# A three-stage kernel with smaller first-layer units, masks behind a chunk's products, and an earlier weight load

## The reference

```python
for t in range(S):
    new_re = ar * S_re - ai * S_im
    new_im = ar * S_im + ai * S_re
    S_re, S_im = (new_re + kv, new_im)                       # kv = k[t] outer v[t]
    y[:, :, t] = np.einsum('bhd,bhde->bhe', q[:, :, t], S_re)
...
h = x @ w_in;  g = h * np.clip(h + 3.0, 0.0, 6.0) / 6.0;  x = g @ w_out
...
h = x @ w_in;  g = np.maximum(h, 0.0) + alpha * np.minimum(h, 0.0);  out = g @ w_out
```

## Time and profile before

| | us |
|---|---|
| median of 3 executions (1058.98 to 1059.59) | 1059.11 |
| the profiled execution | 1056.71 |
| its span, first to last instruction | 1055.0 |
| TensorE busy in the span | 964.5 (91%) |
| VectorE busy | 615.8 (58%) |
| ScalarE busy | 485.1 (46%) |
| GpSimd busy | 303.5 (29%) |
| TensorE's clock, mean share of full speed | 0.979 |

### The profile page before, as it was taken

The page is one execution under the profiler, slowest core; times in us unless marked ns, Lnnn a source line. Parts: engine busy times, 40 slices in busy tenths (PEclk is TensorE's granted clock), DMA queues, the critical chain, the costliest instruction groups (busy, mean ns, idle before and its releaser), DMA issues.

```text
span 1055.0 us, 16550 instructions
## 1 busy us (share of the span) xinstructions
PE 964.5 (91%) x6306; PEld 845.2 (80%) x6306; DVE 615.8 (58%) x1050; ACT 485.1 (46%) x848; POOL 303.5 (29%) x259
## 2 busy tenths in 40 slices
PE   0468888999999998889999999999999999999997
PEld 0468887999999998888787888888888888888886
DVE  6578967888888888667772244453343433433332
ACT  6467666776667776556652444221121211211111
POOL 2048311222222222111222233332332333333232
PEclk9998989999999999889999999999999999999999
DMA  6460432334323333323221701001010010010000
GB/s 199 127 177 24 99 97 69 97 77 107 98 70 91 85 88 98 90 72 78 67 56 37 269 31 60 1 1 60 1 45 16 1 60 1 22 38 1 30 1 31
DMA packets 79616, 70.46 MB, mean 67 GB/s; under 512 B 32560, under 2 KB 76592, under 8 KB 79152
## 3 DMA queue, kind: packets, MB, share of 16 engines
q1 hardware_dynamic: 78896, 68.80, 23.9%
q10 hardware_dynamic: 640, 0.59, 0.2%
HBM read 40.90 MB, written 9.44 MB: 48 GB/s over the span
## 4 chain that ended last, share of the span: by engine, by line
PE 70%; DVE 10%; SPq 8%; DMA 4%; ACT 4%; issue 2%; ACTq 0%; DVEq 0%
PE op L1176 11%; PE op L1177 10%; PE op L1178 10%; PE hp L1177 10%; PE hp L1176 10%; PE hp L1178 10%; SPq L397 4%; SPq L400 4%; DMA st<-prod 3%; PE gp L1143 2%; DVE t_fb L837 2%; PE yp L1143 2%; DVE t_fb L825 2%; PE yp L1164 2%; DVE t_fb L843 1%
## 5 line engine op out<-in xcount | busy, mean ns | idle before, releaser
L519 POOL TENSOR_TENSOR g_lo<-gated,g_hi 128x512 fp32r<-128x512 f32 (+2 forms) x224 | 266.9, 1191 | 689.7 <-ACT g_hi L626 689.7
L626 ACT ACTIVATE g_hi<-gated 128x512 fp32r<-128x512 f32 (+2 forms) x224 | 126.4, 564 | 313.1 <-DVE gated L903 284.2
L899 DVE TENSOR_SCALAR gate<-hp,alpha_sb 128x512 f32<-128x512 f32 x96 | 72.1, 751 | 240.4 <-PE hp L1178 240.4
L1176 PE MATMUL op<-g_hi,wb_hi 128*128 128x384 f32 (+2 forms) x384 | 137.8, 359 | 4.6 <-POOL g_lo L519 4.6
L1176 PE MATMUL hp<-x_hi,wa_hi 128*128 128x384 f32 (+2 forms) x384 | 133.1, 347 | 5.8 <-DVE gated L888 4.4
L888 DVE SCALAR_TENSOR_TENSOR gated<-gate,hp 128x384 f32<-128x384 f32 (+2 forms) x128 | 70.4, 550 | 110.2 <-ACT gate L619 109.4
L1178 PE MATMUL op<-g_hi,wb_lo 128*128 128x384 f32 (+2 forms) x384 | 132.0, 344 | 0.0
L1177 PE MATMUL op<-g_lo,wb_hi 128*128 128x384 f32 (+2 forms) x384 | 131.8, 343 | 0.0
L1178 PE MATMUL hp<-x_hi,wa_lo 128*128 128x384 f32 (+2 forms) x384 | 130.1, 339 | 0.0
L1177 PE MATMUL hp<-x_lo,wa_hi 128*128 128x384 f32 (+2 forms) x384 | 130.1, 339 | 0.0
L619 ACT ACTIVATE gate<-hp,half 128x384 f32<-128x384 f32 (+2 forms) x128 | 73.2, 573 | 106.5 <-PE hp L1178 106.4
(11 more groups left out here) (107 smaller groups left out, 1712.1 us busy)
## 6 DMA issues: line engine op xcount, KB each, us to landing
st<-prod SPq DMA_DIRECT2D x92, 145.1 KB, 2.9
a_sb<-a_in SPq DMA_DIRECT2D x24, 288.0 KB, 4.0
qk_sb<-qk_in SPq DMA_DIRECT2D x24, 288.0 KB, 3.6
v_pad<-v_in SPq DMA_DIRECT2D x24, 192.0 KB, 3.8
x_raw<-x SPq DMA_DIRECT2D x6, 768.0 KB, 5.5
out<-out_sb SPq DMA_DIRECT2D x6, 768.0 KB, 3.8
st<-prod SPq DMA_DIRECT2D x96, 32.2 KB, 1.9
wa_raw<-w_in SPq DMA_DIRECT2D x6, 512.0 KB, 8.1
```

The source lines that it names most:

```text
L519: pool.tensor_tensor(g_lo[:, at, 0:wide], gated[:, at * UT:at * UT + wide], g_hi[:, at, 0:wide].bitcast(F32), ALU.subtract).then_inc(glo_d ...
L626: act.activation(g_hi[:, at, 0:wide], gated[:, at * UT:at * UT + wide], ACT.Copy).then_inc(ghi_done, 1)
L899: dve.tensor_scalar(gate[:, at], hp[:, n % 2, 0:wide], 0.0, alpha_sb[:, m:m + 1], ALU.min, ALU.mult).then_inc(gate_done, 1)
L1176: pe.matmul(acc, lhs[0], rhs[0], start=start, stop=False)
```

## The change

It has four parts.

1. `SIZES` becomes (2, 2, 2, 3, 3, 3, 3, 3, 3): nine units for eight, none wider than 384 columns, 16 items more. Positions have 5, 6 or 8 items.
2. The steps are A to G. On VectorE the forward scan moves to A ahead of the item's gate, backward scan and products go to B, the masks to C (the same item as B in positions of 5 and 6 items, the next in those of 8), low part and state to E. On TensorE the outputs and the new state move from B to D, one item later in positions of 5 and 6 items, two in those of 8. On ScalarE `copy_ends` moves to A, `x_high` to E, ratios and later steps keep their item or nearly.
3. In the prologue SyncE issues load 6 (the first of the second matrix) and q and k of chunk 1 ahead of the row copies of chunk 0; `W_ORDER` has all three second blocks of the first matrix ahead of the first block of the second.
4. In the four items without a chunk, gates and high parts alternate, `angle(3)` comes one gate later, and VectorE makes the second gate ahead of the decay parts of chunk 3.

```diff
-SIZES = (2, 2, 3, 3, 3, 3, 4, 4)
+SIZES = (2, 2, 2, 3, 3, 3, 3, 3, 3)
...
-STEPS = {4: (0, 1, 1, 2, 3, 3), 5: (0, 1, 1, 2, 3, 4), 6: (0, 1, 1, 2, 3, 4), 8: (0, 1, 2, 3, 5, 6)}
+STEPS = {5: (0, 1, 1, 2, 3, 3, 4), 6: (0, 1, 1, 2, 3, 3, 4), 8: (0, 1, 2, 3, 4, 5, 6)}
...
-W_ORDER = (A_BLOCKS[0] + B_BLOCKS[0:1] + A_BLOCKS[1] + B_BLOCKS[1:4] + A_BLOCKS[2] + B_BLOCKS[4:6] + A_BLOCKS[3]
+W_ORDER = (A_BLOCKS[0] + A_BLOCKS[1] + B_BLOCKS[0:4] + A_BLOCKS[2] + B_BLOCKS[4:6] + A_BLOCKS[3]
...
             load_a(2)
+            load_w(6)
+            load_qk(1)
             stack(0)
-            load_qk(1)
             load_a(3)
-            load_w(6)
             stack(1)
...
-            gate_of(0)
-            gate_of(1)
-            high(0)
-            angle(3)
-            high(1)
+            for n in range(2):
+                gate_of(n)
+                high(n)
             squares(4)
             for n in range(ALONE):
                 gate_of(n + GSTEP)
                 high(n + GSTEP)
+                if n == 0:
+                    angle(3)
...
             state(1)
+            gate1(1)
             decay_parts(3)
-            gate1(1)
+            gate1(2)
             mags(4)
-            for n in range(ALONE):
+            for n in range(1, ALONE):
                 gate1(n + GSTEP)
...
                     phases(c1)
                     fractions(c1)
+                    forward(c1)
                 gate1(n + GSTEP)
-                if "A" in steps:
+                if "B" in steps and c1 is not None:
+                    backward(c1)
+                    products(c1)
+                if "C" in steps:
                     mask(c0, 0)
                     mask(c0, 1)
-                if "B" in steps and c1 is not None:
-                    forward(c1)
-                    backward(c1)
-                if "C" in steps and c1 is not None:
-                    products(c1)
-                if "D" in steps:
+                if "E" in steps:
                     x_low(c0)
...
-                if "B" in steps:
+                if "D" in steps:
                     outputs(c0)
```

More of the change, by code:

```diff
@@ L120, in places @@
         items = items_of(s)
-        count = min(max(len(items), 4), 8)
-        steps = STEPS[min(STEPS, key=lambda k: (k < count, k))] if count not in STEPS else STEPS[count]
         for i, n in enumerate(items):
-            yield ("".join(x for x, at in zip("ABCDEF", steps) if at == i), n, chunk_at(s), chunk_at(s + 1),
+            yield ("".join(x for x, at in zip("ABCDEFG", STEPS[len(items)]) if at == i), n, chunk_at(s), chunk_at(s + 1),
                    chunk_at(s + 2), chunk_at(s + 3))
@@ L445, in _ @@
                         load_qk(c2)
-                if "E" in steps and c1 is not None:
+                if "F" in steps and c1 is not None:
                     load_v(c1)
-                if "F" in steps:
+                if "G" in steps:
                     c4 = chunk_at(c0 + 4)
@@ L718, in _ @@
                         copy_k(c0, 1)
-                    if c1 is not None:
-                        copy_ends(c1)
                     if c2 is not None:
                         logs(c2)
-                if "D" in steps:
+                if "D" in steps and c2 is not None:
+                    inverses(c2)
+                if "E" in steps:
                     x_high(c0)
-                    if c2 is not None:
-                        inverses(c2)
-                if "E" in steps and c3 is not None:
+                if "F" in steps and c3 is not None:
                     squares(c3)
-                if "F" in steps and c2 is not None:
+                if "G" in steps and c2 is not None:
                     angle(c2)
@@ L993, in _ @@
                         state(c0)
-                if "E" in steps and c2 is not None:
+                if "F" in steps and c2 is not None:
                     residue(c2)
```

1 line of the change is left out of this document (added).

## The result

The changed kernel takes 1048.26 us (median of 4 runs, 1043.73 to 1049.45), beside 1059.05 for the kernel before on the same chip: a ratio of 0.989, 95% interval 0.986 to 0.992. The profiled execution took 1048.43 us with a span of 1046.7, so 8.3 us less than the profiled one of before; all that follows is told against that span.

The account below looks back on a forecast made before the run. TensorE was taken as the nearly always busy engine, losing time to row-copy waits and low clock, with a prologue ahead. Terms -7.5 + 3.3 + 3.4 - 43.6 + 30.9 + 2 = -11.5 gave 1047 us, within 1028 to 1063.

Parts of the forecast that it names:

- Prologue, -7.5: Before chunk 1: the earlier load ends ScalarE's wait, so chunk 1's scores start at 43.0 instead of 50.56, -7.5 us.
- Lone items, 0: Four items without a chunk: the reorder only shifts work within busy ScalarE, so it costs nothing.
- First unit, +3.3: First unit's two positions: masks come later and VectorE waits a round trip for outputs, copy and state, +3.3 us.
- Narrower units, +3.4: From item 15 to the second layer: sixteen items more in narrower units make the matmuls longer, 373 against 370, +3.4 us.
- Waits going, -43.6: Chunk 4 to second layer: row-copy waits, small gaps and low-clock work go with the units of four chunks, -43.6 us.
- Mask waits, +30.9: Chunk positions before the second layer: TensorE's outputs now wait for VectorE's masks, 30.9 us in all.
- The extra 0.4 us of lag: Ten positions of width 384: the forward scan delays item 0's gate, so the mask wait is about 1.35 us, not 0.9.
- Clock, +2: Behind the first positions' mask waits of over 3 us: TensorE's clock falls low, +2 us.
- a clock of 1.00 from chunk 6 on: Sign that the forecast is right: TensorE's granted clock reads 1.00 from chunk 6 on.
- Rival 1: Units of width 384: masks come in time, so TensorE does not wait for them, 1028 us; chance 0.16.
- Rival 2: Gain eaten early: prologue only -4, first unit +8, three-chunk unit at width 256 +3 worse, 1058 us; chance 0.12.
- Rival 3: Every position: the round trip makes VectorE the bound, 2.6 us per position instead of 1.25, 1067 us; chance 0.16.

Follow-up runs that it names:

- The prologue alone: Kernel before with only the second matrix's first load, chunk 1's q and k and the split order moved as in the change: 1049.5 us, ratio 0.992.
- part 4 undone: Changed kernel with the old order of gates, high parts and third angle in the lone items: 1047.4 us; likewise with masks and outputs back: 1022.7.
- three more units of 2 chunks: Changed kernel with masks and outputs moved back, and sizes 2, 2, 2, 2, 2, 2, 3, 3, 3, 3: 1024.1 us, ratio 0.968.
- the masks home: Changed kernel with masks back at the first item behind the gate: 1022.9 us with outputs moved back too, 1021.7 with outputs kept late.
- the sizes alone: Kernel before with only the new unit sizes (2, 2, 2, then six units of 3 chunks): 1035.8 us, ratio 0.979.
- the order alone: Kernel before with all engines' new steps, old sizes, prologue and lone items, plus a four-item row; last chunk's copies one item earlier: 1088.4 us, ratio 1.028.
- the masks and outputs back and the old sizes: Changed kernel with masks and outputs moved back and the old unit sizes, plus a step-table row for four items: 1035.9 us, ratio 0.979.

## Why the prediction came out right, and where its steps were off

Forecast 1047 within 1028 to 1063; it is 1048.3, a change of -10.8 for -11.5. The mechanism, row waits out and mask waits in, is in the trace and in the experiments. Its terms, on the profiled spans (sum -11.5 foretold, -8.3 in the trace):

- **Prologue, -7.5.** 50.56 to 43.08 is -7.48. ScalarE's 9.51 us wait is gone, and SyncE's copies of chunk 1 are what comes next, as said. They end at 41.77 instead of 41.0 and the scores follow 1.3 us later instead of 2, two small errors that cancel. The prologue alone gave 7.9.
- **Lone items, 0.** The stretch between the starts of chunks 1 and 2 is 1.5 us longer (31.41 to 32.90): TensorE now waits 3.30 us at 69 us for GpSimd's `wb_lo`, in place of 4.45 us for the gate at 72 us. Its idle time falls from 8.01 to 5.76 us; what grows is the time at the low clock (0.90 over the stretch instead of 0.95). The step looked at ScalarE and the next gate alone, not at GpSimd. The order makes this wait, not the early start: with part 4 undone everything starts as early and the wait is absent. Nothing of it is left in the time of either pair of kernels, since the first unit gives it back.
- **First unit, +3.3.** 47.46 to 51.77, +4.3. In chunk 2's position the masks end 16.5 us after the scores begin (92.45-75.98), as foretold (98.5-81.97), and the masks hold TensorE 6.40 us at 92.50 and 3.42 at 116.72.
- **Narrower units, +3.4.** Its own working gives 2.9 (372.9 less 370.0), not 3.4. Not measured by itself. An estimate: TensorE's busy time in the stretch, less what the low clock costs (see Clock), is 496.20-12.8 = 483.4 us before and 492.89-8.2 = 484.7 after, so +1.3. With three more units of 2 chunks the net loss is 1.2 us, inside the spread of runs.
- **Waits going, -43.6.** Right for the changed kernel: no row wait is left. The margin was put too wide, though. The copies start at +10.07, as foretold (367.97-357.90), but take 8.56 us to issue instead of 7.75 (in the position of the earlier trace rows it was 8.05, from 363.85 to 371.90), so they land at about 20.6 instead of 19.8, below 21.6. With the masks home they start at +10.70 and land at 21.4, and with the sizes alone, where the forward row comes late, eight row waits stay, 13.0 us. The 43.6 itself was 2.9 too much: TensorE's idle time in the stretch before is 27.9 us and the low clock costs 12.8 there, 40.7 in all.
- **Mask waits, +30.9.** 22.9 measured. The three in the positions of chunks 6, 7 and 8 were sized well (2.94, 3.31, 3.48 against 3.4 each). The fourteen in width 384 are 13.2, not 18.8: twelve are 0.80 to 0.87 and two are 1.76 and 1.39. The extra 0.4 us of lag that I gave ten positions did not come: ScalarE's gate stands at +5.52 as before (363.42-357.90), since VectorE idles before the gate and the early forward row falls into that time. The two positions of eight items have none.
- **Clock, +2.** Too little. The sign "a clock of 1.00 from chunk 6 on" did not come: from 174.33 to 244.65 (chunks 6 to 8) the granted clock is 0.88, and it is 1.00 from chunk 9 on. About half clock was granted in three pieces, from 187.5, 208.0 and 231.5 us on, beside the mask waits of 2.94, 3.31 and 3.48. They cost 8.2 us of the stretch (12.8 before), an estimate: busy time times what the clock lacks to 1.00, summed over pieces of half a microsecond. The forecast held 2; this used up most of what the mask waits left over.

So the stretch came out at -6.6 against -7.3 by errors of opposite sign: masks 8.0 too dear, low clock 6.2 too cheap, and 2.5 in what is left (2.9 of waits that were not there to go, 1.7 of other idle time, mostly the two waits for `g_lo` above, and -2.1 in the matmuls). That the total hit so closely is in part luck. **Rival 1** (masks in time, 1028) did not happen, but its argument holds, that little else is late: with the masks in another place the time is 1022. **Rival 2** came in small part: the first unit cost 4.3 and not 8, the three positions in width 256 lost what the low clock took, and the prologue's gain was whole. **Rival 3** did not: VectorE is busy 254.47 of 326.01 us, 0.78.

What the prediction did not say is which part pays. With the new sizes and prologue the order and the lone items make 1048.3 of 1028.3, 20 us (18 by the ratios 0.989 and 0.972); with the old sizes it is about 30, in a form that has its own row for four items; and the one line of sizes brings 21.6 by itself. That sum could have been made from the same rows: the 30.9 of mask waits stood in it as the order's, and nothing in it asked what the order bought.

## What to carry to other kernels

Put a short step that another engine waits for into a gap in which its own engine waits anyway, here the masks between two gates; behind a 5 us chain it cost its consumer a wait in every position of five or six items, and moving it earlier by one step gives the wait to someone else unless it falls into such a gap. Where a unit's work is spread over the next unit's chunks, keep neighbouring units alike: the items of a unit of three, spread over the four chunks of the next, gave positions shorter than the chunk's own chain, and those are where TensorE waited. When a change has parts, time each alone: here one part lost more than half of what the others won.

## What the runs showed of the hardware

Waits of TensorE of about 3 to 5 us were mostly followed by a low granted clock, even where TensorE was then busy without a gap. In the changed kernel, outputs that waited 2.94 us at 186.38 are followed by:

```profile
187.90:194.70 6.80, 6.80 (x38) 6.80 (x38) 2.78 (x7) 2.12 (x6) 0.73 (x2) 0.53 0.46 115
```

that is, mostly the lower level of 1.2 instead of 2.4 GHz for 6.8 us, 3.2 us of work lost (0.47 x 6.80), more than the wait. Shorter waits in every position had no such effect: from chunk 9 to 23 the clock is 1.00 with fourteen of them, 0.80 to 1.76 us. The length of the wait alone does not decide it. In the order alone a wait of 3.48 us that ended at 169.08 was followed by clock 1.00 until 173, and one of 3.14 at 424.97 by 1.00 until 433; with the masks and outputs back and the old sizes, 2.69 us at 409.94 left it at 1.00 until 418, while 1.99 at 452.89 was followed by 0.52 from 453.0 to 456.5. The Trainium skill (TensorE: Matmul & The Clock Gate, What's actually happening) describes a clock gated by recent activity; the direction agrees, and the trace's number is the 0.53 above. That the wait causes the low clock was not tested by itself; it is how they stand in the traces, and in the kernel with more units of two chunks the clock is 1.00 from chunk 4 to 9, where no wait is longer than 1.04 us.
